# First-layer weights in five chunks: the 64 remaining features as high and low parts on both row halves

## The chip, the cores and the metric

The kernel runs on one core of a Trainium2 chip. The metric is the device time in microseconds, the median of several executions; lower is better. Inputs are made from a fixed seed and are float32.

## What is computed

An mLSTM-like recurrence over 4 batches, 8 heads, 768 steps and a head size of 40 is followed by two pairs of feed-forward layers on the 3072 x 320 result. Cut to what matters:

```python
x = attn_out.transpose(0, 2, 1, 3).reshape(B * S, H * D)     # 3072 x 320
def _moe_ref(x, w_in, w_out):        # w_in 320 x 2048, w_out 2048 x 320
    h = x @ w_in
    return np.maximum(0.01 * h, h) @ w_out
def _moe2_ref(x, w_in, w_out):       # the same shapes
    h = x @ w_in
    return (h * np.cos(h)) @ w_out
```

The change is in `h = x @ w_in`, in both pairs. Both products are made in three terms of rounded operands: with x = x_hi + x_lo and w = w_hi + w_lo, the kernel sums w_hi x_hi, w_hi x_lo and w_lo x_hi (for some features w_lo x_lo too).

## The kernel before

**Tiling.** The 3072 rows are 8 blocks of 384 (`BLOCKS`, `BLOCK`), half a batch each, three units of 128 rows in a block. The hidden size of 2048 is 16 tiles of 128 (`FT`). For each block and tile TensorE makes a first product (`first_product`, line 635 of the profile's numbering `L635`: eight matmuls of 128x384) and, three tiles later (`LAG`), a second product (`second_product`, lines 647 to 649: nine of 128x320). The first pair of layers runs over all 8 blocks, then the second pair.

**Stages in time.** Up to 36 us the first three units of the recurrence are computed with nothing beside them. From there on `slot(row, i)` of each engine is called for each tile i by `over_the_row`; into the slots of a block the steps of the next three units are put (`UNIT_SLOTS`, and `FIRST_SLOTS` for block 0: scores in slots 3, 7 and 11, probabilities one slot later, outputs two, read three, transposition four). Each engine executes its own list strictly in order, and the order is written out by hand; engines meet through semaphores (`wait_ge`, `then_inc`). From 480 us on the second pair of layers runs, with nothing of the recurrence beside it.

**The features.** 320 features are two chunks of 128 and a remainder of 64 (`REM`). The remainder fills a chunk of its own by standing twice, on partitions 0 to 63 and 64 to 127. In x (`xT`, five chunks) chunks 0 and 1 are the high parts of the full chunks, 3 and 4 their low parts; chunk 2 has the remainder's high part on the lower half of the partitions and its low part on the upper half. In the weights (`w_in`, six chunks) 0 to 2 are high parts and 3 to 5 low parts, the remainder's being the same on both halves. So the pair (weights 2, x 2) gives w_hi x_hi + w_hi x_lo of the remainder and (weights 5, x 2) gives w_lo x_hi + w_lo x_lo.

**Making the parts of x.** TensorE transposes a unit, ScalarE copies all three chunks in rounded form (`round_turned`), VectorE subtracts (`split_turned`, lines 1185 and 1186, called by `x_lo` for the first pair of layers and in `slot` under `turn2` for the second, into `stage`, which goes to DRAM and comes back).

**Making the parts of the weights.** SyncE loads raw pieces of two tiles (`load_raw_in`, two buffers, so that piece k waits for the splits of piece k-2), ScalarE rounds all three chunks (`split_in_hi`, `swap_in_hi`), and the rest is a subtraction: on GpSimd for pieces 0 and 1 (line 1447), on VectorE for pieces 2 to 7 (line 1283) in slots 1, 2, 5, 6, 9 and 10 of block 0 (`LATE_IN`). For the second pair of layers, GpSimd does it tile by tile during block 7 (`swap_in_lo`, line 1470), each followed by the output weights' rest (`swap_out_lo`, line 1476).

**The order around the start.** GpSimd: `split_in_lo(0)`, `second_columns()` (gate steps, lines 1435 and 1438, which wait for VectorE's scan `gate_decays(1)`, line 1051), `split_out_lo(0)` (line 1482), `split_in_lo(1)`, `split_out_lo(1)`, then unit 3. SyncE: raw piece 2 of both weights, the second of which waits for `split_out_lo(0)`, then the decays of units 3 and 4, then raw piece 3. VectorE at the end of the first stage: `normalised(0, 2)`, `gate_decays(1)`, `x_lo(0, 0)`, `outputs(0, 2)`, `x_lo(0, 1)`, `x_lo(0, 2)`.

Of the kernel before, what the change touches and what calls it, by code (L numbers as in the profile page):

```python
# [20 lines left out]
F32 = mybir.dt.float32  # L21
F32R = mybir.dt.float32r
ALU = mybir.AluOpType
ACT = mybir.ActivationFunctionType

P = 128
# [4 lines left out]
BLOCK = SEQ // HALVES  # L31
BLOCKS = BATCH * HALVES
TILES = BLOCK // P
DM, FF = HEADS * HD, 2048
FT = FF // P
REM = DM - 2 * P
SUB, SUBS = 64, 2
# [11 lines left out]
PIECES = 8  # L49
RAW_IN, RAW_OUT = 2, 2  # L50
# [3 lines left out]
PT = FT // PIECES  # L54
# [21 lines left out]
def build(nc, qk, q3, kvo, ig, fg, w1i, w1o, w2i, w2o, out, g_dram, e_dram, x2_dram):  # L76
    ctx = ExitStack()
    with ctx:
        def sb(name, shape, dt=F32):
            return ctx.enter_context(nc.sbuf_tensor(name, shape, dt))  # L80
# [4 lines left out]
        def sem(name):  # L85
            return ctx.enter_context(nc.semaphore(name))


        w_in = sb("w_in", [P, 6, FF], F32R)
        w_out = sb("w_out", [P, 2, FT, DM], F32R)  # L90
        raw_in = sb("raw_in", [P, RAW_IN, 3, PT * P])
        raw_out = sb("raw_out", [P, RAW_OUT, PT, DM])

        xT = sb("xT", [P, 2, 5, BLOCK], F32R)
        stage_f = sb("stage", [P, 5, BLOCK])
        stage = stage_f[:, :, :].bitcast(F32R)
        g_hi = sb("g_hi", [P, RING, BLOCK], F32R)
        g_lo = sb("g_lo", [P, RING, BLOCK], F32R)
# [63 lines left out]
        colb_done = sem("colb_done")  # L162
        win_hi = sem("win_hi")
        win_lo = sem("win_lo")
        wout_hi = sem("wout_hi")
        wout_lo = sem("wout_lo")
        arg_done = sem("arg_done")
# [91 lines left out]

        def half_cols(k):  # L260
            return slice(k * BLOCK, (k + 1) * BLOCK)

        def splits(k):

            return k + 1 if k < PIECES else PIECES + (k - PIECES + 1) * PT
# [80 lines left out]
        @block.sync  # L346
        def _(sp):
            sp.dma_start(f_s[:, half_cols(0)], fg[:, half_cols(0)]).then_inc(gates_in, 16)

            def wait_count(semaphore, count):  # L350
# [65 lines left out]

            load_qk(0, 0)
            sp.dma_start(f_s[:, half_cols(1)], fg[:, half_cols(1)]).then_inc(gates_in1, 16)
            sp.dma_start(i_s[:, half_cols(1)], ig[:, half_cols(1)]).then_inc(gates_in1, 16)
            load_kvo(0, 0)  # L420
            load_q3(0, 0)
# [119 lines left out]
        def _(pe):  # L541
# [88 lines left out]

            def first_product(bank, x, j):
                w = lambda k: w_in[:, k, j * P:(j + 1) * P]
                order = [(0, 0), (0, 3), (3, 0), (1, 1), (1, 4), (4, 1), (2, 2), (5, 2)]
                for n, (a, k) in enumerate(order):
                    last = nc.tensor.matmul(bank[:, 0:BLOCK], w(a), x[:, k, :], start=(n == 0), stop=(n == 7))  # L635
                last.then_inc(h_done, 1)
# [25 lines left out]
            def slot(row, i):  # L662
# [3 lines left out]
                if exists(row, i) and not row.in_mlp2(i):  # L666
                    if j == 0:
                        pe.wait_ge(xT_done, row.block(i) * TILES + TILES)
                    if row.starts(0, i) and j % PT == 0:
                        pe.wait_ge(win_lo, j // PT + 1)  # L670
                    pe.wait_ge(max_done, row.tile(i) - 1 + H_FREE)
                    first_product(h_bank[i % 2], xT[:, row.half(i)], j)
                elif exists(row, i):
                    if j == 0:
                        pe.wait_ge(x2_in[row.half(i)], row.block(i) * 8 - 8 * row.half(i) - 48)
                    if row.starts(BLOCKS, i):
                        pe.wait_ge(win_lo, PIECES + j + 1)
                        if j < H_FREE:
                            pe.wait_ge(max_done, row.tile(i) - 1 + H_FREE)
                    pe.wait_ge(prod_done, row.tile2(i) - 3 + PROD_FREE)  # L680
                    first_product(ring_bank[i % 4], xT[:, row.half(i)], j)
# [333 lines left out]
        def _(dve):  # L1015
            tt = nc.vector.tensor_tensor
# [164 lines left out]
            def split_turned(dst, bank, t):  # L1181

                r = slice(t * P, (t + 1) * P)
                src = bank[:, 0:3 * P].rearrange("p (a t) -> p a t", a=3)
                tt(dst[:, 3:5, r], src[:, 0:2, :], dst[:, 0:2, r].bitcast(F32), ALU.subtract)
                return tt(dst[REM:P, 2, r], src[REM:P, 2, :], dst[REM:P, 2, r].bitcast(F32), ALU.subtract)  # L1186

            def x_lo(b, c, dst):
                dve.wait_ge(xh_done, unit(b, c) + 1)
                split_turned(dst, turn_bank(b, c), c % TILES).then_inc(xT_done, 1)  # L1190
# [5 lines left out]
            def slot(row, i):  # L1196
# [41 lines left out]
                if t is not None:  # L1238
                    dve.wait_ge(x2_hi, (row.block(i) - 1) * TILES + t + 1)
                    split_turned(stage, x_bank, t).then_inc(x2_split, 1)  # L1240
                if row.starts(0, i) and i in LATE_IN:
                    split_in_lo(LATE_IN[i])
# [36 lines left out]
            def split_in_lo(k):  # L1279
                dve.wait_ge(win_hi, k + 1)  # L1280
                dve.wait_ge(win_lo, k)
                c = slice(k * PT * P, (k + 1) * PT * P)
                tt(w_in[:, 3:6, c], raw_in[:, k % RAW_IN, :, :], w_in[:, 0:3, c].bitcast(F32), ALU.subtract).then_inc(win_lo, 1)

            gate_maxima(1)
            first_probs(0)
# [27 lines left out]
        def _(pool):  # L1314
# [129 lines left out]
            def split_in_lo(k):  # L1444
                pool.wait_ge(win_hi, k + 1)
                c = slice(k * PT * P, (k + 1) * PT * P)
                nc.gpsimd.tensor_tensor(w_in[:, 3:6, c], raw_in[:, k % RAW_IN, :, :], w_in[:, 0:3, c].bitcast(F32),
                                        ALU.subtract).then_inc(win_lo, 1)

            def unit_weights(b, c):  # L1450
                if c == 0:
# [14 lines left out]
            def swap_in_lo(j):  # L1466

                pool.wait_ge(win_hi, PIECES + j + 1)
                k, c = PIECES + j // PT, slice(j * P, (j + 1) * P)
                nc.gpsimd.tensor_tensor(w_in[:, 3:6, c], raw_in[:, k % RAW_IN, :, j % PT * P:(j % PT + 1) * P],  # L1470
                                        w_in[:, 0:3, c].bitcast(F32), ALU.subtract).then_inc(win_lo, 1)

            def swap_out_lo(j):
                pool.wait_ge(wout_hi, PIECES + j + 1)
# [21 lines left out]
            second_inputs()  # L1496
            gated(0, 1)
            split_in_lo(0)
            second_columns()
            split_out_lo(0)  # L1500
            split_in_lo(1)
            split_out_lo(1)
            unit_weights(0, 3)
# [31 lines left out]
            for i in range(SWAP_IN, 2 * FT + 2):  # L1535
                if i >= FT + 2:
                    g_rest(0, i - FT - 2)
                if i < SWAP_IN + FT:
                    swap_in_lo(i - SWAP_IN)
                if SWAP_OUT <= i < SWAP_OUT + FT:  # L1540
                    swap_out_lo(i - SWAP_OUT)
# [58 lines left out]
```

## Time and profile before

| | |
|---|---|
| median of 3 executions | 835.13 us (834.86 to 835.85) |
| the profiled execution | 836.9 us, span 835.1 us |
| TensorE busy | 98% of the span |
| VectorE busy | 76% |
| ScalarE busy | 56% |
| GpSimd busy | 41% |
| mean granted clock of TensorE | 0.996 |
| DMA | 70.26 MB, mean 84 GB/s |

How to read it: the span runs from the first to the last instruction of the profiled execution, and that execution's own time is a little more. Busy shares are means over stages with different limits: a busy TensorE is where little can be hidden, and the idle time of the other engines costs nothing in itself. "Idle before, releaser" names what ended an engine's wait by the semaphores. The names: PE is TensorE, PEld its weight loads, DVE VectorE, ACT ScalarE, POOL GpSimd, SP SyncE.

### The profile page before, as it was taken

The numbers are of one execution on the slowest core, as the hardware profiler recorded it, in microseconds if no ns is written. First come the engines' busy times: TensorE is split into PE (matmuls) and PEld (weight loads), VectorE is DVE, ScalarE is ACT, GpSimd is POOL, SyncE is SP. The second block draws the span as 40 slices with busy tenths as digits, with TensorE's granted clock in tenths as the row PEclk, the third lists the DMA queues.
The fourth block names the chain that finished last, engine by engine and source line by source line (L and its number), as shares of the span: only waits on it lengthen the run. The fifth ranks groups of instructions, "written<-read, shape, count | busy, mean of one in ns | idle before, by whom it ended". The sixth has DMA issues, their size and how long they took to land.

```text
span 835.1 us, 18267 instructions
## 1 busy us (share of the span) xinstructions
PE 815.9 (98%) x6953; PEld 784.8 (94%) x6953; DVE 633.1 (76%) x1377; ACT 465.3 (56%) x1033; POOL 339.9 (41%) x350
## 2 busy tenths in 40 slices
PE   8789999999999999999999999999999999999997
PEld 6678899999999999999999999999999999999997
DVE  7679677677677866777853588888888888888886
ACT  5245443433433434334336687767776767777776
POOL 5656534343333433433316643333333333333332
PEclk9989999999999999999999999999999999999999
DMA  9555522423444324235023410302020202020000
GB/s 300 174 151 149 172 78 79 126 78 82 129 134 131 89 79 125 79 91 183 1 96 108 121 75 2 119 2 72 1 72 1 72 1 71 1 72 1 20 5 25
DMA packets 37292, 70.26 MB, mean 84 GB/s; under 512 B 3544, under 2 KB 24408, under 8 KB 37208
## 3 DMA queue, kind: packets, MB, share of 16 engines
q1 hardware_dynamic: 36708, 68.86, 26.7%
q8 instruction: 55, 0.90, 0.5%
q10 hardware_dynamic: 500, 0.26, 0.1%
q14 instruction: 29, 0.24, 0.1%
HBM read 57.11 MB, written 11.99 MB: 83 GB/s over the span
## 4 chain that ended last, share of the span: by engine, by line
PE 90%; DVE 4%; ACT 1%; DMA 1%; issue 1%; POOL 1%; SPq 1%; DVEq 0%; POOLq 0%; ACTq 0%
PE h L635 32%; PE acc L647 13%; PE acc L649 13%; PE acc L648 13%; PE s L635 10%; PE x L613 2%; PE s L593 2%; PE s L577 2%; PE s L605 2%; PE s L558 1%; DVE g_lo L1194 1%; DMA raw_in<-w1i 1%; DVE kvo_s L1073 1%; DMA eG_b<-e_dram 1%; ACT t_f L791 0%
## 5 line engine op out<-in xcount | busy, mean ns | idle before, releaser
L635 PE MATMUL h<-xT,w_in 128*128 128x384 f32 x1536 | 306.5, 341 | 0.5 <-DVE xT L1186 0.5
L635 PEld LDWEIGHTS h<-xT,w_in 128*128 128x128 f32 x1536 | 266.5, 188 | 3.6 <-DVE xT L1186 0.6
L791 ACT ACTIVATE t_f<-h 128x384 f32<-128x384 f32 x192 | 94.4, 492 | 291.9 <-PE h L635 291.8
L647 PE MATMUL acc<-w_out,g_hi 128*128 128x320 f32 x768 | 242.1, 315 | 2.2 <-POOL g_lo L1533 1.8
L649 PE MATMUL acc<-w_out,g_lo 128*128 128x320 f32 x768 | 237.5, 309 | 0.0
L648 PE MATMUL acc<-w_out,g_hi 128*128 128x320 f32 x768 | 236.2, 308 | 0.0
L1533 POOL TENSOR_TENSOR g_lo<-g_f,g_hi 128x384 fp32r<-128x384 f32 x127 | 130.2, 1025 | 211.9 <-ACT g_hi L791 211.9
L1207 DVE TENSOR_TENSOR g_f<-h,t_f 128x384 f32<-128x384 f32 x128 | 71.2, 556 | 105.7 <-ACT t_f L791 105.7
L647 PEld LDWEIGHTS acc<-w_out,g_hi 128*128 128x128 f32 x768 | 144.6, 188 | 4.6 <-POOL g_lo L1533 2.0
L648 PEld LDWEIGHTS acc<-w_out,g_hi 128*128 128x128 f32 x768 | 144.7, 188 | 0.0
L649 PEld LDWEIGHTS acc<-w_out,g_lo 128*128 128x128 f32 x768 | 144.3, 188 | 0.0
L791 ACT ACTIVATE g_hi<-g_f 128x384 fp32r<-128x384 f32 (+1 forms) x258 | 132.8, 515 | 1.6 <-DVE g_f L1227 1.0
L1219 DVE SCALAR_TENSOR_TENSOR r_f<-t_f,r_f 128x384 f32<-128x384 f32 x127 | 115.0, 906 | 4.4
L1380 POOL TENSOR_TENSOR Cm<-C,own 80x328 f32<-80x328 f32 x44 | 36.4, 830 | 170.2 <-DVE C L1175 140.5
L635 PE MATMUL s<-xT,w_in 128*128 128x384 f32 x512 | 100.8, 338 | 0.0
L1194 DVE TENSOR_TENSOR g_lo<-g_f,g_hi 128x384 fp32r<-128x384 f32 x128 | 95.7, 748 | 0.0
L635 PEld LDWEIGHTS s<-xT,w_in 128*128 128x128 f32 x512 | 89.7, 188 | 0.0
L1215 DVE TENSOR_SCALAR t_f<-t_f 128x384 f32<-128x384 f32 x127 | 46.8, 368 | 45.9 <-ACT t_f L791 45.8
L937 ACT ACTIVATE r_f<-r_f,half_pi 128x384 f32<-128x384 f32 x127 | 78.6, 619 | 4.1
L935 ACT ACTIVATE r_f<-r_f 128x384 f32<-128x384 f32 x127 | 65.5, 515 | 0.0
L1073 DVE RECIPROCAL kvo_s<-kvo_s 128x160 f32<-128x160 f32 x48 | 55.1, 1148 | 4.6 <-ACT kvo_s L791 4.5
L791 ACT ACTIVATE t_f<-s 128x384 f32<-128x384 f32 x64 | 31.6, 493 | 41.6 <-PE s L635 41.6
(150 smaller groups left out, 792.5 us busy)
## 6 DMA issues: line engine op xcount, KB each, us to landing
qk_s<-qk SPq DMA_DIRECT2D x24, 512.0 KB, 3.8
kvo_s<-kvo SPq DMA_DIRECT2D x24, 484.0 KB, 5.2
x_dram<-stage SPq DMA_DIRECT2D x8, 960.0 KB, 6.0
xT<-x_dram SPq DMA_DIRECT2D x8, 960.0 KB, 4.9
D<-g_dram SPq DMA_DIRECT2D x42, 128.0 KB
qe<-q SPq DMA_DIRECT2D x24, 160.0 KB, 5.5
out<-x SPq DMA_DIRECT2D x24, 160.0 KB, 1.8
eG_b<-e_dram SPq DMA_DIRECT2D x42, 80.0 KB
```

The costliest lines, as they stand in the source:

```text
L635: last = nc.tensor.matmul(bank[:, 0:BLOCK], w(a), x[:, k, :], start=(n == 0), stop=(n == 7))
L647: nc.tensor.matmul(acc[t][:, 0:DM], g_hi[:, s, r], w_out[:, 0, j, :], start=(j == 0), stop=False)
L648: nc.tensor.matmul(acc[t][:, 0:DM], g_hi[:, s, r], w_out[:, 1, j, :], start=False, stop=False)
L649: nc.tensor.matmul(acc[t][:, 0:DM], g_lo[:, s, r], w_out[:, 0, j, :], start=False, stop=(j == FT - 1)).then_inc(out_done, 1)
L791: copy = lambda o, i, **k: nc.scalar.activation(o, i, ACT.Copy, **k)
L935: nc.scalar.activation(r, r, ACT.Abs).then_inc(fold_done, 1)
L937: nc.scalar.activation(r, r, ACT.Sin, bias=half_pi[:, 0:1], scale=-1.0).then_inc(sin_done, 1)
L1073: nc.vector.reciprocal(o, o).then_inc(sig_done, 1)
L1194: tt(g_lo[:, i % RING, :], g_f[:, i % RING, :], g_hi[:, i % RING, :].bitcast(F32), ALU.subtract).then_inc(lo_done, 1)
L1207: tt(g_f[:, i % RING, :], h_bank[i % 2][:, 0:BLOCK], t_f[:, i % 2, :], ALU.max).then_inc(max_done, 1)
L1219: nc.vector.scalar_tensor_tensor(r, k, -TWO_PI_LO, r, ALU.mult, ALU.add).then_inc(red_done, 1)
L1533: nc.gpsimd.tensor_tensor(g_lo[:, s, :], g_f[:, s, :], g_hi[:, s, :].bitcast(F32), ALU.subtract).then_inc(lo_done, 1)
```

## The change

`w_in` has five chunks in place of six, `xT`, `stage` and `x2_dram` six in place of five. x now holds high parts in 0 to 2 and low parts in 3 to 5, the remainder's on both halves of the partitions. In the weights, chunk 2 has the high part of the remainder on one half and the low part on the other: for even tiles the low part is on the upper half (`rest_rows`), for odd tiles on the lower. So (weights 2, x 2) gives w_hi x_hi + w_lo x_hi, and (weights 2, x 5), in place of (weights 5, x 2), gives the products with x_lo. `split_turned` is one subtraction of three chunks. Each split of weights is a subtraction of two chunks and, for each tile, one of a half chunk in place. On GpSimd these wait for one another by a new semaphore `win_step`. ScalarE's steps are the same.

```diff
-        w_in = sb("w_in", [P, 6, FF], F32R)
+        w_in = sb("w_in", [P, 5, FF], F32R)
-        xT = sb("xT", [P, 2, 5, BLOCK], F32R)
-        stage_f = sb("stage", [P, 5, BLOCK])
+        xT = sb("xT", [P, 2, 6, BLOCK], F32R)
+        stage_f = sb("stage", [P, 6, BLOCK])
+        def rest_rows(j):
+            return slice(SUB * (1 - j % 2), SUB * (2 - j % 2))
@@ first_product
-                order = [(0, 0), (0, 3), (3, 0), (1, 1), (1, 4), (4, 1), (2, 2), (5, 2)]
+                order = [(0, 0), (0, 3), (3, 0), (1, 1), (1, 4), (4, 1), (2, 2), (2, 5)]
@@ split_turned (VectorE)
-                tt(dst[:, 3:5, r], src[:, 0:2, :], dst[:, 0:2, r].bitcast(F32), ALU.subtract)
-                return tt(dst[REM:P, 2, r], src[REM:P, 2, :], dst[REM:P, 2, r].bitcast(F32), ALU.subtract)
+                return tt(dst[:, 3:6, r], src, dst[:, 0:3, r].bitcast(F32), ALU.subtract)
@@ split_in_lo (VectorE)
-                tt(w_in[:, 3:6, c], raw_in[:, k % RAW_IN, :, :], w_in[:, 0:3, c].bitcast(F32), ALU.subtract).then_inc(win_lo, 1)
+                for j in range(PT):
+                    r, b = rest_rows(j), slice((k * PT + j) * P, (k * PT + j + 1) * P)
+                    tt(w_in[r, 2, b], raw_in[r, k % RAW_IN, 2, j * P:(j + 1) * P], w_in[r, 2, b].bitcast(F32), ALU.subtract)
+                tt(w_in[:, 3:5, c], raw_in[:, k % RAW_IN, 0:2, :], w_in[:, 0:2, c].bitcast(F32), ALU.subtract).then_inc(win_lo, 1)
@@ split_in_lo (GpSimd)
-                nc.gpsimd.tensor_tensor(w_in[:, 3:6, c], raw_in[:, k % RAW_IN, :, :], w_in[:, 0:3, c].bitcast(F32),
-                                        ALU.subtract).then_inc(win_lo, 1)
+                nc.gpsimd.tensor_tensor(w_in[:, 3:5, c], raw_in[:, k % RAW_IN, 0:2, :], w_in[:, 0:2, c].bitcast(F32),
+                                        ALU.subtract).then_inc(win_step, 1)
+                pool.wait_ge(win_step, PT * k + 1)
+                for j in range(PT):
+                    r, b = rest_rows(j), slice((k * PT + j) * P, (k * PT + j + 1) * P)
+                    nc.gpsimd.tensor_tensor(w_in[r, 2, b], raw_in[r, k % RAW_IN, 2, j * P:(j + 1) * P], w_in[r, 2, b].bitcast(F32),
+                                            ALU.subtract).then_inc(win_step if j == 0 else win_lo, 1)
+                    if j == 0:
+                        pool.wait_ge(win_step, PT * k + 2)
@@ swap_in_lo (GpSimd)
-                nc.gpsimd.tensor_tensor(w_in[:, 3:6, c], raw_in[:, k % RAW_IN, :, j % PT * P:(j % PT + 1) * P],
-                                        w_in[:, 0:3, c].bitcast(F32), ALU.subtract).then_inc(win_lo, 1)
+                r, b = rest_rows(j), slice(j % PT * P, (j % PT + 1) * P)
+                nc.gpsimd.tensor_tensor(w_in[:, 3:5, c], raw_in[:, k % RAW_IN, 0:2, b], w_in[:, 0:2, c].bitcast(F32),
+                                        ALU.subtract).then_inc(win_step, 1)
+                pool.wait_ge(win_step, PT * RAW_IN + j + 1)
+                nc.gpsimd.tensor_tensor(w_in[r, 2, c], raw_in[r, k % RAW_IN, 2, b], w_in[r, 2, c].bitcast(F32),
+                                        ALU.subtract).then_inc(win_lo, 1)
+                pool.wait_ge(win_lo, PIECES + j + 1)
@@ kernel
-    x2_dram = nc.dram_tensor("x2_dram", [BLOCKS, P, 5, BLOCK], F32, kind="Internal").ap()
+    x2_dram = nc.dram_tensor("x2_dram", [BLOCKS, P, 6, BLOCK], F32, kind="Internal").ap()
```

## Rows read from the trace of the kernel before

**Rows 1.** The page, part 1: TensorE's busy time, share of the span, instructions.

```profile
PE 815.9 (98%) x6953; PEld 784.8 (94%) x6953; DVE 633.1 (76%) x1377; ACT 465.3 (56%) x1033; POOL 339.9 (41%) x350
```

**Rows 2.** Windows: stretch, length, busy us by engine, granted clock, DMA share, GB/s.

```profile
52.00:54.00 2.00, 2.00 (x18) 1.85 (x19) 2.00 (x3) 0.00 (x0) 0.68 (x1) 0.50 0.14 27
...
57.40:57.60 0.20, 0.20 (x3) 0.20 (x2) 0.20 (x1) 0.20 (x1) 0.00 (x0) 0.83 0.00 0
...
300.00:400.00 100.00, 99.81 (x1036) 93.51 (x1035) 73.38 (x185) 41.16 (x99) 33.55 (x35) 1.00 0.38 116
```

**Rows 3.** TensorE's waits: who waited for whom, us in total, times, longest.

```profile
PE s L577 <- DVE D L1081: 4.5, 2, 3.4
...
PE x L613 <- DVE xT L1186: 0.4, 2, 0.2
```

**Rows 4.** The chain that ended last, 31 to 53 us: start, us, what.

```profile
31.87 0.85 DVE t_f L1051
32.79 0.99 POOL stage L1435
...
41.12 6.27 DMA raw_in<-w1i
...
48.30 0.96 DVE w_in L1283
...
51.91 1.38 PE s L577 x16
```

**Rows 5.** Timeline, TensorE, 45 to 47 us: start, length, engine, line, operation.

```profile
45.07 0.31 PE L649 MATMUL acc<-w_out,g_lo 128*128 128x320 f32 x1
...
45.22 0.31 PE L647 MATMUL acc<-w_out,g_hi 128*128 128x320 f32 x1
...
45.36 0.31 PE L648 MATMUL acc<-w_out,g_hi 128*128 128x320 f32 x1
...
45.51 1.38 PEld L635 LDWEIGHTS h<-xT,w_in 128*128 128x128 f32 x8
```

**Rows 6.** Timeline, VectorE and GpSimd, 29 to 34 us.

```profile
29.78 1.80 POOL L1447 TENSOR_TENSOR w_in<-raw_in,w_in 128x768 fp32r<-128x768 f32 x1
...
31.78 0.94 DVE L1051 TENSOR_TENSOR_SCAN t_f<-r_f,stage 32x384 f32<-32x384 f32 x1
32.64 0.39 DVE L1185 TENSOR_TENSOR xT<-x,xT 128x256 fp32r<-128x256 f32 x1
...
33.04 0.29 DVE L1186 TENSOR_TENSOR xT<-x,xT 64x128 fp32r<-64x128 f32 x1
...
33.37 0.18 DVE L1145 TENSOR_TENSOR x<-acc,kvo_s 128x24 f32<-128x24 f32 x1
```

**Rows 7.** Groups by line and shape: busy us, mean ns; idle before and releaser.

```profile
L1207 DVE TENSOR_TENSOR g_f<-h,t_f 128x384 f32<-128x384 f32 x128 | 71.2, 556 | 105.7 <-ACT t_f L791 105.7
...
L1470 POOL TENSOR_TENSOR w_in<-raw_in,w_in 128x384 fp32r<-128x384 f32 x16 | 16.4, 1024 | 29.4 <-ACT w_in L791 29.4
```

**Rows 8.** Timeline, VectorE and TensorE, 65 to 72 us.

```profile
65.78 2.60 DVE L1194 TENSOR_TENSOR g_lo<-g_f,g_hi 128x384 fp32r<-128x384 f32 x1
...
71.06 0.81 PE L577 MATMUL s<-kvo_s,kw 64*80 64x82 f32 x16 [1.14 <-DVE D L1081]
```

**Rows 9.** Timeline, GpSimd and VectorE, 42 to 46 us.

```profile
42.31 1.06 POOL L1351 TENSOR_TENSOR D<-D,colb 128x512 f32<-128x512 f32 x1 [2.35 <-DMA eG_b<-e_dram]
...
42.53 1.66 DVE L1283 TENSOR_TENSOR w_in<-raw_in,w_in 128x768 fp32r<-128x768 f32 x1
...
43.52 1.82 POOL L1356 TENSOR_TENSOR D<-D,hide 128x512 f32<-128x512 f32 x1
```

**Rows 10.** Timeline, GpSimd, 466 to 470 us, in the exchange of weights.

```profile
466.35 1.03 POOL L1470 TENSOR_TENSOR w_in<-raw_in,w_in 128x384 fp32r<-128x384 f32 x1 [0.86 <-ACT w_in L791]
...
467.34 0.87 POOL L1476 TENSOR_TENSOR w_out<-raw_out,w_out 128x320 fp32r<-128x320 f32 x1
```

**Rows 11.** The page, part 6: DMA issues, KB each, us to landing.

```profile
x_dram<-stage SPq DMA_DIRECT2D x8, 960.0 KB, 6.0
```

More of the change, by code:

```diff
@@ L164, in build @@
         win_lo = sem("win_lo")
+        win_step = sem("win_step")
         wout_hi = sem("wout_hi")
```

## The prediction
> **What bounds the kernel now.** I read the page first. TensorE is busy for 815.9 of 835.1 us [rows 1], so only what TensorE waits for, or what changes the pace of its own instructions, can move the time. The windows come next: from 300 to 400 us it is busy for 99.81 of 100 us at full clock [rows 2]. All that it loses is at the start, before the second layer products are in full flow, and at the very end. The list of TensorE's waits says who is to blame [rows 3]: 4.5 us in two places behind VectorE's `D` (the decayed scores), the longest 3.4 us, and 0.4 us in two places behind the low halves of x, line 1186. The chain that ended last tells how the first of these comes about [rows 4]. A scan on VectorE at 31.87 us releases GpSimd's gate steps at 32.79; behind them in GpSimd's order stands the rest of the first output weights, which lets SyncE go on to the loads of the decays, and only then, at 41.12, to the load of first-layer piece 3. That lands 6.27 us later, ScalarE rounds it, VectorE takes its rest at 48.30 (line 1283), and behind it, in VectorE's own order, come a maximum, a rest, a reciprocal and the product `D`, for which TensorE waits until 51.91. [...]
>
> **TensorE's own work.** Each of the 256 first-layer tiles keeps eight matmuls of 128x384. The last one was (weights 5, x 2) and is (weights 2, x 5). Nothing is removed and no shape changes, so I cost it at nothing. The only new thing is that the last two matmuls of a tile load the same weights. The trace has this already in the second layer: from line 649 to 647 the weights change and the step is 0.15 us, from line 647 to 648 they stay and it is 0.14 us [rows 5]. These are the same within the rounding.
>
> **The low halves of x (48 times, lines 1185 and 1186).** Two VectorE instructions become one. Before, they run from 32.64 to the next start at 33.37, 0.73 us [rows 6]. The one that takes their place is a 128x384 difference with one source in PSUM, as line 1207, 556 ns [rows 7]. The scan before them starts its successor 0.08 us before its own end (31.78 + 0.94 against 32.64) [rows 6], so the step should be 0.48 us: 0.25 us saved to the next instruction, and 0.33 + 0.40 - 0.56 = 0.17 us to the semaphore. TensorE waits for this in two places, in full 0.4 us, the longest 0.2 [rows 3]: 0.17 us each, together -0.35 us (bounds 0 and -0.4). The start of the first tile at 36.07 also comes earlier, but that gain flows into the 3.4 us wait behind it and is worth nothing.
>
> **The rests of the weights on VectorE (six pieces, line 1283).** One 128x768 instruction becomes two of 64x128 and one of 128x512. From 556 ns for 384 [rows 7] and 0.96 us for 768 [rows 4] an element costs 1.05 ns and the start 0.15 us; so 512 takes 0.69 us, and 64x128 takes 0.29 us, which is also what line 1186 shows for 64x128 [rows 6]. If each overlaps its successor by 0.08 us, the three take 0.21 + 0.21 + 0.61 = 1.03 us against 0.88, +0.15. Line 1186, on the upper half of the partitions, overlaps neither way (0.40 us from start to start for its neighbour of 0.39, then 0.33 for 0.29) [rows 6]; if both small ones behave so, it is 0.33 + 0.33 + 0.61 = 1.27, +0.39. I take +0.25, between these ends that lie near each other. This stands in the chain once, for the piece at 48.30. [...]
>
> **The rests on GpSimd at the start (pieces 0 and 1, line 1447).** One of 128x768, 1.80 us [rows 6], becomes 128x512, a wait on its own end, 64x128, a wait, 64x128. From 1024 ns for 384 [rows 7] an element costs 2.02 ns and the start 0.25 us: 1.28 + 0.51 + 0.51 us. A wait of GpSimd for its own instruction costs 0.15 us (42.31 + 1.06 against 43.52) [rows 9]. That is 2.6 us in place of 1.8, and piece 0 runs from 29.78 to 32.4. GpSimd has nothing to do before 32.79, so in itself this is hidden. But the scan that opens the chain starts at 31.78 and reads two tensors of SBUF [rows 6]. Such VectorE instructions and GpSimd's exclude each other in this trace: line 1283 at 42.53 takes 1.66 us instead of 0.96 beside GpSimd's `D` steps, and GpSimd's at 43.52 takes 1.82 for the same 512 elements for which 1.28 was worked out [rows 9]; line 1194 at 65.78 takes 2.60 us instead of some 0.55 [rows 8]. The second small one would start at 31.9, on top of the scan. If it waits for the scan, it runs until 33.2 and the gate steps start then instead of at 32.79; if the scan waits for it, the scan ends 0.5 us later. Both give about +0.4 us on the chain. Bounds: 0, if the scan is not touched, and +0.6. I take +0.40. Who waits: the gate steps, the output weights behind them, SyncE's queue and the load at 41.12. Piece 1 starts behind that chain and ends at some 39.2 us, when SyncE needs it only at 41.5: hidden. [...]
>
> **The second wait, 1.14 us at 71.06.** Ahead of it stand, on VectorE, a split of weights, line 1194 with its 2.60 us behind GpSimd, the x split and a reciprocal [rows 8]. The x split gives -0.25 us. The weight split has the blocked stretch after it as cover. Bounds: -1.14, if GpSimd and VectorE take turns better so that the wait goes away, and +1.3, if one of the three new instructions waits for one more GpSimd instruction (1.3 us is the price of 512 elements). I take -0.25.
>
> **The exchange of weights (16 tiles, line 1470).** Each 1.03 us becomes 128x256 (0.77) + 0.15 + 0.51 + 0.15 us = 1.6 us; with the output weights of 0.87 us it makes 2.5 us in a period of 2.7 (0.86 idle, then 0.99 to the next start, then 0.87) [rows 10]. [...] Its weights are needed a whole block later, so I cost it at 0; if GpSimd fell behind by 0.2 us in each of the 16, it would reach the next block's `g_lo` 3 us late, of which the lag of three tiles (8 us) hides all.
>
> **Transfers.** The stores and loads of x2 carry 6/5 of 960 KB, 1152 KB, landing about 1.2 us later than 6.0 us [rows 11]; each has more than a third of a block to land in. Nothing.
>
> **The sum** against the profiled execution (span 835.1, own time 836.9): +0.40 + 0.25 - 0.25 - 0.35 = +0.05 us. That execution lies 1.8 us above the median of 835.13, and the difference is put on the median: 835.2 us. The bounds are -1.14 - 0.4 + 0 + 0.15 = -1.4 us and 0.6 + 0.39 + 1.3 - 0 = +2.3 us.
>
> **Rivals.** [...] The first chain takes its upper ends (+0.99) and the second wait its own (+1.3, one of the three instructions of the split of weights ahead of it queues behind one more of GpSimd), while the two waits for x give back 0.35: +1.9 us, 837.1. It decides from the point where at least 1 us is lost at the second wait. For it speaks the 2.60 us of line 1194, against it that the stretch at 65.78 is blocked until 68.38 already, so that a delay of the split vanishes in it. 12 in 100. (b) Faster by the clock: the low-clock stretch after the wait costs half of 57.5 - 51.9, that is 2.8 us. If the wait moves so that the fall no longer comes, the time is 832.4. Against it: the wait gets longer in my sum, by 0.65 us and by TensorE's earlier start. 4 in 100. (c) Faster by the taking of turns: the second wait goes (-1.14), and the chain is not touched (0.15): 835.13 - 1.14 - 0.35 + 0.15 = 833.8, still within 0.2%, 8 in 100. [...] 3 in 100. (e) The longer wait also makes the low-clock stretch longer: half as long again is +1.4 us, with the first chain's +0.65 and -0.6 after it 836.6: within 0.2%, 6 in 100.
>
> **How the numbers follow.** The forecast itself has 67 in 100. 0.2% is 1.67 us, about what a measurement of this kernel can tell from no change. Within it lie the forecast, (c) and (e), 81 in 100; slower is (a), 12; faster are (b) and (d), 7. The range takes in (c) and (e) and most of (a): 833.6 to 837.0.
>
> **What would show it.** The gate step at 32.79 should start at 33.1 to 33.3 and the load of piece 3 at 41.5; the three instructions of the piece at 48.7 should take 1.0 to 1.3 us to the next start; TensorE's first long wait should end near 52.5, the second be shorter by a quarter of a microsecond, and the two waits for x's low halves be gone. TensorE's steps of 0.172 and 0.145 us should be as before. The forecast is wrong if these steps move, if the clock falls in another place, or if a wait appears in the blocks after 100 us.

## The result and the profile after

The changed kernel takes 837.36 us (median of 13), the one before 835.84 us beside it; the ratio is 1.0023, with a 95% interval of 1.0012 to 1.0033. It is slower by 1.9 us (1.0 to 2.8). I had forecast 835.2 us, that is no change against the 835.13 of before, and a range up to 837.0: a loss of 1.9 us was not in it. Of the 2.2 us between 835.2 and 837.36 some 0.7 belong to the kernel before, whose median is higher in this larger set of executions.

The two profiled executions hardly differ in span, 835.3 against 835.1 us, and this has to be cleared up first. The windows from 46 to 60 us, before first and after second, show why (columns as in [rows 2]):

```profile
46.00:60.00 14.00, 10.61 (x100) 9.86 (x100) 9.97 (x24) 6.03 (x12) 4.77 (x5) 0.76 0.56 153
```

```profile
46.00:60.00 14.00, 11.59 (x125) 10.62 (x126) 11.19 (x30) 6.48 (x14) 5.93 (x7) 0.88 0.62 161
```

Both lose clock at TensorE's long wait near 50 us (before is granted 0.50 from 51.0 to 57.4), but the execution of before that was profiled loses twice as much of it (granted 0.76 against 0.88). In time that is 3.4 us lost (0.24 of 14) against 1.7 (0.12 of 14). The other traces below show 0.76, 0.88 or 1.00 there, and neither the edits nor the length of the wait orders them. Executions of one and the same kernel differ by some 3 us, and this is part of it. So I compare stretches that lie behind it, from one landmark of TensorE's order to the next. The landmarks are waits that both traces have. After:

```profile
69.05 0.80 PE L582 MATMUL s<-kvo_s,kw 64*80 64x82 f32 x16 [0.64 <-DVE D L1086]
...
73.64 0.79 PE L598 MATMUL s<-Cm,qe 80*64 80x82 f32 x16 [0.88 <-POOL Cm L1387]
...
79.82 0.55 PE L618 MATMUL x<-ident,x 128*128 128x128 f32 x3 [0.45 <-DVE x L1154]
...
87.01 0.52 PE L582 MATMUL s<-kvo_s,kw 64*80 64x82 f32 x8 [1.80 <-DVE D L1086]
...
96.12 0.55 PE L618 MATMUL x<-ident,x 128*128 128x128 f32 x3 [0.99 <-DVE x L1154]
```

And the last of these landmarks before:

```profile
95.06 0.55 PE L613 MATMUL x<-ident,x 128*128 128x128 f32 x3 [0.99 <-DVE x L1149]
```

The first row answers to 71.06 in [rows 8]. From there to the last landmark it is 27.07 us after and 24.00 us before, 3.07 us more. From the last landmark to the end of the span it is 739.2 us after and 740.0 before, 0.9 us less. Together +2.2 us. Up to the first of these landmarks the changed kernel is 2.0 us ahead, 1.7 of it by the lesser loss of clock; the 0.3 us that are left bring the sum to +1.9 us, the measured loss. The new thing is the wait of 1.80 us at 87.01, where before had none worth naming.

What leads to it stands in the timeline of VectorE and GpSimd. Before, in the slots 9 to 12 of block 0:

```profile
80.01 1.42 POOL L1356 TENSOR_TENSOR D<-D,hide 128x512 f32<-128x512 f32 x1
81.38 1.45 POOL L1368 TENSOR_TENSOR kw<-kvo_s,colb 128x320 f32<-128x320 f32 x1
82.79 1.61 POOL L1362 TENSOR_TENSOR qe<-qe,eG_b 80x512 f32<-80x512 f32 x1
```

```profile
80.86 1.38 DVE L1283 TENSOR_TENSOR w_in<-raw_in,w_in 128x768 fp32r<-128x768 f32 x1
...
82.63 0.61 DVE L1194 TENSOR_TENSOR g_lo<-g_f,g_hi 128x384 fp32r<-128x384 f32 x1
```

After:

```profile
78.83 1.41 POOL L1363 TENSOR_TENSOR D<-D,hide 128x512 f32<-128x512 f32 x1
80.21 0.77 POOL L1375 TENSOR_TENSOR kw<-kvo_s,colb 128x320 f32<-128x320 f32 x1
80.94 1.95 POOL L1369 TENSOR_TENSOR qe<-qe,eG_b 80x512 f32<-80x512 f32 x1
82.85 1.56 POOL L1501 TENSOR_TENSOR w_out<-raw_out,w_out 128x640 fp32r<-128x640 f32 x1
```

```profile
79.80 1.32 DVE L1289 TENSOR_TENSOR w_in<-raw_in,w_in 64x128 fp32r<-64x128 f32 x2
81.05 0.68 DVE L1290 TENSOR_TENSOR w_in<-raw_in,w_in 128x512 fp32r<-128x512 f32 x1
...
82.12 2.70 DVE L1198 TENSOR_TENSOR g_lo<-g_f,g_hi 128x384 fp32r<-128x384 f32 x1
84.75 0.55 DVE L1190 TENSOR_TENSOR xT<-x,xT 128x384 fp32r<-128x384 f32 x1
...
86.27 0.68 DVE L1086 TENSOR_TENSOR D<-s,D 128x256 f32<-128x256 f32 x2
```

Read them as turns at one door; in the expectations I call it the port. What the rows show is who waits and for how long, not what the two engines share. The door concerns VectorE's instructions with two sources in SBUF: `g_f` (line 1207 before, 1211 after), with one source in PSUM, takes 0.54 to 0.56 us each of the 128 times, also at 81.65 in the middle of `qe`. Before, the single weight instruction is served behind GpSimd's `D`, `kw` waits for it (1.45 us in place of some 0.75), then the rest of g (`g_lo`, line 1194 before and 1198 after) is served between `kw` and `qe`. After, the first small one is served behind `D`, then GpSimd's `kw` comes at once (0.77 us), then the second small one and the large one, and it is `qe` that waits (1.95 us). The rest of g now asks at 82.12, while `qe` runs, and it isn't served at the end of `qe` at 82.89 but only at the end of the output weights' rest at 84.41. It takes 2.70 us instead of 0.61, and behind it in VectorE's order stand the x split, a reciprocal and the product `D` for which TensorE waits.

TensorE's own steps are as forecast. After, at full clock:

```profile
48.02 0.31 PE L652 MATMUL acc<-w_out,g_hi 128*128 128x320 f32 x1
48.16 0.31 PE L653 MATMUL acc<-w_out,g_hi 128*128 128x320 f32 x1
48.31 0.31 PE L654 MATMUL acc<-w_out,g_lo 128*128 128x320 f32 x1
```

The steps are those of [rows 5]; a matmul of the first layer takes 341 ns in the mean on the pages of both kernels. From 300 to 400 us TensorE is busy for 99.95 us with 1038 instructions against 1036 [rows 2].

### The profile page after: what moved, and what is told of

It reads as the page before. It is cut to its first block, busy times and chain, and to the rows that moved or that the text cites. A ratio compares the mean times of both kernels' runs of the same rounds, so it can differ in the third digit from the quotient of the medians.

```text
span 835.3 us, 18267 instructions
## 1 busy us (share of the span) xinstructions
PE 816.5 (98%) x6953; PEld 784.9 (94%) x6953; DVE 630.2 (75%) x1341; ACT 465.0 (56%) x1033; POOL 343.7 (41%) x370
## 4 chain that ended last, share of the span: by engine, by line
PE 90%; DVE 5%; ACT 2%; issue 1%; DMA 1%; POOL 0%; DVEq 0%; POOLq 0%; ACTq 0%
PE h L640 32%; PE acc L652 13%; PE acc L654 12%; PE acc L653 12%; PE s L640 10%; PE x L618 2%; PE s L598 2%; PE s L582 2%; PE s L610 2%; PE s L563 1%; DVE kvo_s L1078 1%; DVE g_lo L1198 1%; DMA eG_b<-e_dram 1%; DVE g_f L1211 1%; DMA raw_in<-w1i 0%
## 5 line engine op out<-in xcount | busy, mean ns | idle before, releaser
L1198 DVE TENSOR_TENSOR g_lo<-g_f,g_hi 128x384 fp32r<-128x384 f32 x128 | 97.9, 765 | 0.0
```

The lines of the kernel that those rows point to most:

```text
L1198: tt(g_lo[:, i % RING, :], g_f[:, i % RING, :], g_hi[:, i % RING, :].bitcast(F32), ALU.subtract).then_inc(lo_done, 1)
```

## The experiments

Every figure in us against the kernel before is the ratio's, on runs side by side on one chip.

**The parts of the change, one at a time.** VectorE's weight splits alone:

```diff
-                tt(w_in[:, 3:6, c], raw_in[:, k % RAW_IN, :, :], w_in[:, 0:3, c].bitcast(F32), ALU.subtract).then_inc(win_lo, 1)
+                for j in range(PT):
+                    r, b = rest_rows(j), slice((k * PT + j) * P, (k * PT + j + 1) * P)
+                    tt(w_in[r, 2, b], raw_in[r, k % RAW_IN, 2, j * P:(j + 1) * P], w_in[r, 2, b].bitcast(F32), ALU.subtract)
+                tt(w_in[:, 3:5, c], raw_in[:, k % RAW_IN, 0:2, :], w_in[:, 0:2, c].bitcast(F32), ALU.subtract).then_inc(win_lo, 1)
```

> Only the VectorE weight splits of the change: pieces 2 to 7 take two instructions of 64x128 and one of 128x512 in place of one of 128x768. x keeps five chunks, the last matmul of a tile repeats (weights 2, x 2), chunk 5 goes unread, so the products of the remainder are not the reference's. Theory 1 (port queue): 1.5 to 2.8 us slower than before, and in the trace a new wait of TensorE of 1 us or more near 87 us behind line 1194's rest, itself of 2.5 us or more. Rival (the three instructions cost only their own length, +0.25 us on the first chain): 0.2 to 0.4 us slower and no new wait between 80 and 90 us.

Measured: 839.61 us against 835.55, ratio 1.0055 (1.0040 to 1.0070), +4.6 us. The wait near 87 us is 2.28 us long and from the first landmark to the last it is 27.06 us. Theory 1 holds for the wait and the rest of g ahead of it, 2.71 us, not for the price, of which I had expected 1.5 to 2.8 us. The part costs more than the whole change, by five executions; 3.1 of the 4.6 us lie between the landmarks, and where the rest lies was not settled.

The GpSimd weight splits alone (`split_in_lo` and `swap_in_lo` of GpSimd as in the diff of the change):

> Only the GpSimd weight splits of the change: pieces 0 and 1 at the start and the 16 tiles of the exchange are cut into their parts with the waits between. VectorE's splits stay single, x keeps five chunks, the last matmul of a tile repeats (weights 2, x 2), chunk 5 goes unread, so the products of the remainder are not the reference's. Theory 1: within 0.5 us of before; the scan at 31.8 us is lengthened by 0.2 us at most 0.5, which reaches the first long wait, and nothing is seen near 480 us. Rival (the start chain carries the loss): 1 us or more slower, with the first long wait of TensorE ending 1 us later.

Measured: 835.16 against 835.55 us, ratio 0.9999 (0.9988 to 1.0010). From landmark to landmark 23.99 us, to the end 740.0 us: nothing. The chain at the start doesn't carry the loss.

The x part alone (`split_turned` in one instruction, six chunks; the weights' rests in single instructions into chunks 0 to 2):

> Only the x part of the change: x in six chunks, one VectorE subtraction of 128x384 for two, 1152 KB to and from DRAM. The weights' rests are single subtractions of three chunks as before, but take the place of the high parts in chunks 0 to 2, and the eight matmuls of a tile use these three chunks only, so the products are not the reference's. Theory 1 (the whole loss lies in VectorE's three small weight instructions): 0.9 to 1.9 us faster than before, with TensorE's waits for the low halves of x (0.2 us at 207 and 318 us) gone and 0.9 to 1.0 us less between 96 us and the end, as the changed kernel has it. Rival (x gives only the 0.35 us of my sum): 0.2 to 0.5 us faster.

Measured: 834.60 against 835.68 us, ratio 0.9992 (0.9978 to 1.0005). The interval holds both no gain and 1.8 us; the trace says more:

```profile
70.23 0.81 PE L582 MATMUL s<-kvo_s,kw 64*80 64x82 f32 x16 [0.66 <-DVE D L1086]
...
74.80 0.79 PE L598 MATMUL s<-Cm,qe 80*64 80x82 f32 x16 [0.86 <-POOL Cm L1384]
...
94.60 0.55 PE L618 MATMUL x<-ident,x 128*128 128x128 f32 x3 [0.99 <-DVE x L1154]
```

To the end of the span (833.7) it is 739.1 us from the last landmark, 0.9 less than before, as in the changed kernel. The first row has the wait of 1.14 us [rows 8] shortened by 0.5 us, and the second shows where that goes: the next wait grows from 0.37 to 0.86 us. Larger transfers cost nothing.

**Which piece.** VectorE's splits as in w_vector_only, but for the last piece (`if k < 7:`), and then for the last piece alone (`if k == 7:`):

> As w_vector_only, but the last piece (slot 10 of block 0) has its single 128x768 subtraction back; the products of the remainder are not the reference's. Theory 1 (one starved rest at slot 10 carries most of the loss: GpSimd takes the port for the small instructions' sake one instruction earlier, and the rest of tile 9 then waits through two of GpSimd's in a row): the wait of TensorE near 87 us falls from 2.3 to under 0.3 us, and the time from 4.1 to some 1.5 to 2 us above before. Rival (each of the six pieces costs its share by the length of its instructions): the loss falls by a sixth, to some 3.4 us.

Measured: 836.42 against 835.68 us, ratio 1.0010 (1.0001 to 1.0019); 23.93 us between the landmarks, no wait at 83 us. Five pieces in three instructions cost 0.8 us, less than the 1.5 to 2 I had expected, and by difference the sixth 3.8. The stall one unit earlier is still there, 2.71 us for line 1198 at 63.66 as in before at 65.78, and TensorE's second wait is 2.00 us in this trace, whose clock did not fall.

> The kernel before, but VectorE's last piece of weights alone (piece 7, slot 10 of block 0) is taken in three instructions; x keeps five chunks, the last matmul of a tile repeats (weights 2, x 2), so the products of the remainder are not the reference's. Theory 1 (the piece at slot 10 shifts the turn at the port, and one starved rest costs the time): a wait of TensorE of 1.5 to 2.3 us near 87 us, nothing of it at the other pieces, and 2 to 3 us slower than before. Rival (the six pieces add up, or the stall needs the shifts of the pieces before it): 0 to 0.6 us slower and no such wait.

Measured: 838.57 against 835.39 us, ratio 1.0037 (1.0022 to 1.0053), +3.1 us; 26.7 us between the landmarks. Its rows:

```profile
83.29 2.71 DVE L1198 TENSOR_TENSOR g_lo<-g_f,g_hi 128x384 fp32r<-128x384 f32 x1
```

```profile
88.67 0.52 PE L581 MATMUL s<-kvo_s,kw 64*80 64x82 f32 x8 [2.31 <-DVE D L1085]
```

One piece in one slot is the loss. The rival, that pieces add up, has fallen: the other five together cost 0.8 us (0.1 to 1.6) against 3.1 (1.8 to 4.4).

**Fewer small instructions.** The low part on the upper half for every tile, one 64x256 in a piece:

```diff
-            return slice(SUB * (1 - j % 2), SUB * (2 - j % 2))
+            return slice(SUB, P)
@@ VectorE
+                tt(w_in[SUB:P, 2, c], raw_in[SUB:P, k % RAW_IN, 2, :], w_in[SUB:P, 2, c].bitcast(F32), ALU.subtract)
```

> The changed kernel with the low part of the remainder on the upper half for every tile, so that the two small instructions of a piece are one of 64x256: two VectorE instructions in a piece in place of three, two on GpSimd at the start. Theory 1 (each small instruction may queue anew, and shifts GpSimd's turn): the same stall near 87 us, if one small instruction is enough to shift the turn, and then at most 0.5 us faster than the changed kernel; without the stall 2 us faster or more. Rival (number of instructions counts): 0.2 us in each of the pieces on the path, 0.5 us in all.

Measured: 837.16 against 835.68 us, ratio 1.0014 (1.0001 to 1.0027). The stall is there, 2.69 us and a wait of 1.74 us at 87 us. One instruction more than before is enough to shift the turn.

**Opening the door.** GpSimd waits for its own `qe` ahead of the output weights' rest:

```diff
             unit_weights(0, 3)
+            pool.wait_ge(qe_done, 4)
             split_out_lo(2)
@@ and in units 4 and 5 alike
```

> The changed kernel, with one wait more on GpSimd in each of units 3, 4 and 5: for the end of its own product qe, ahead of the output weights' rest, so that GpSimd has an idle moment between the two. Theory 1 (the rest of g on VectorE is starved because GpSimd passes from qe, on 80 partitions, into the next instruction without letting the port go): the 2.6 and 2.7 us instructions of line 1198 near 64 and 82 us fall to 1.6 us or less, the waits of TensorE near 69 and 87 us go, and the time falls by 2 to 3 us, to 0.5 us or more below before. Rival (GpSimd keeps its turn whatever the gap): no change against the changed kernel.

Measured: 835.92 against 835.68 us, ratio 1.0000 (0.9987 to 1.0014), about 1.9 us less than the changed kernel has over before, but not the 0.5 us below before that I had expected. GpSimd and VectorE:

```profile
78.47 1.95 POOL L1369 TENSOR_TENSOR qe<-qe,eG_b 80x512 f32<-80x512 f32 x1
80.50 1.77 POOL L1501 TENSOR_TENSOR w_out<-raw_out,w_out 128x640 fp32r<-128x640 f32 x1
```

```profile
79.65 1.19 DVE L1198 TENSOR_TENSOR g_lo<-g_f,g_hi 128x384 fp32r<-128x384 f32 x1
...
83.36 1.67 DVE L1198 TENSOR_TENSOR g_lo<-g_f,g_hi 128x384 fp32r<-128x384 f32 x1
```

The rest of g asks at 79.65, during `qe`, as in the changed kernel, and is done at 80.84: it enters in the 0.08 us between `qe` and the next. The waits at 69 and 87 us shrink to nothing and 0.31 us. Part of the gain is missing because another wait appears, 1.50 us at 87.98: the next rest of g (second row) now finds the next output weights in its way. The granted clock may take another part: of the twelve executions six have a mean of 0.998 and take 833.3 to 834.9 us, six have 0.991 to 0.994 and take 837.0 to 838.4, so that the median of 835.92 lies between two groups. The kernel before has 0.997 in the mean of its 35, this one 0.996. What takes the clock in the second group wasn't traced.

> The kernel before with the same three waits on GpSimd as in after_gap. Its rest near 66 us takes 2.60 us behind two GpSimd instructions, and TensorE waits 1.14 us at 71 us. Theory 1: this falls to 1.6 us or less, the wait goes, and the time falls by 0.7 to 1.5 us. Rival (the turn at the port does not depend on the gap): no difference.

Measured: 833.92 against 835.39 us, ratio 0.9991 (0.9974 to 1.0007), -0.8 us: not settled by the times. In the trace the rest of g falls from 2.60 us [rows 8] to 1.07, and TensorE has no wait over 0.12 us between 53 and 93 us. The stall was in the kernel before too, at unit 4, and I had read it as given.

> The changed kernel with one small instruction of 64x256 in a piece (as paired2) and the three waits on GpSimd of after_gap. Theory 1: as after_gap or up to 0.4 us faster, since one start less stands in each piece, and 0.5 to 1.5 us below before by the saving on x. Rival (the gap helps only together with a certain place of the small instructions): as paired2.

Measured: 835.79 against 835.39 us, ratio 1.0003 (0.9994 to 1.0012), as after_gap; the 0.5 to 1.5 us below before did not come. Its trace has the same new wait, 1.60 us at 88.38.

**How long the door stays shut behind `qe`.** First `kw` and `qe` in the other order:

```diff
-                keys(b, c)
-                carried(b, c)
+                carried(b, c)
+                keys(b, c)
```

> The changed kernel with GpSimd's kw (128 partitions) and qe (80 partitions) in the other order in every unit, so that the instruction ahead of the output weights' rest is the one on 128 partitions, still with no wait between. [...] Theory 1b (any two GpSimd instructions with no wait between keep the port): the stalls stay, within 0.5 us of the changed kernel.

Measured: 837.86 against 835.39 us, ratio 1.0029 (1.0017 to 1.0041).

```profile
80.92 1.33 POOL L1369 TENSOR_TENSOR qe<-qe,eG_b 80x512 f32<-80x512 f32 x1
82.22 0.72 POOL L1375 TENSOR_TENSOR kw<-kvo_s,colb 128x320 f32<-128x320 f32 x1
82.90 1.56 POOL L1501 TENSOR_TENSOR w_out<-raw_out,w_out 128x640 fp32r<-128x640 f32 x1
```

```profile
80.52 4.08 DVE L1289 TENSOR_TENSOR w_in<-raw_in,w_in 64x128 fp32r<-64x128 f32 x2
84.53 0.68 DVE L1290 TENSOR_TENSOR w_in<-raw_in,w_in 128x512 fp32r<-128x512 f32 x1
```

The time is what theory 1b gives (0.5 us more than the changed kernel, within the noise), the rows are not so simple. I had expected VectorE to be served behind `kw`, since that uses all 128 partitions, and the time to fall by 1.5 to 3 us. It is not: the second small instruction now waits through `qe`, `kw` and the output weights, and ends at 84.61. But theory 1b falls by the rows of before above, where VectorE is served between `kw` and `qe` with no wait between (0.61 us at 82.63). What fits both is that VectorE stays shut out behind `qe` for more than one instruction. So the same order with a wait behind `qe` and none behind `kw`:

```diff
                 carried(b, c)
+                if isinstance(b, int) and b == 0:
+                    pool.wait_ge(qe_done, unit(b, c) + 1)
                 keys(b, c)
```

> after_swap with one wait more in units 3 to 5: GpSimd waits for the end of qe (80 partitions) before kw (128 partitions); between kw and the output weights' rest there is still no wait. [...] Theory 1b (any two GpSimd instructions with no wait between keep the port): the small ones are served in the gap, but the rest of line 1198 waits for kw and the output weights' rest both, 2.2 us or more.

Measured: 835.54 against 835.74 us, ratio 0.9999 (0.9989 to 1.0010), 2.5 us less against before than after_swap.

```profile
79.21 1.33 POOL L1369 TENSOR_TENSOR qe<-qe,eG_b 80x512 f32<-80x512 f32 x1
80.62 1.26 POOL L1375 TENSOR_TENSOR kw<-kvo_s,colb 128x320 f32<-128x320 f32 x1
81.84 1.88 POOL L1503 TENSOR_TENSOR w_out<-raw_out,w_out 128x640 fp32r<-128x640 f32 x1
```

```profile
78.79 1.90 DVE L1289 TENSOR_TENSOR w_in<-raw_in,w_in 64x128 fp32r<-64x128 f32 x2
...
81.68 0.61 DVE L1198 TENSOR_TENSOR g_lo<-g_f,g_hi 128x384 fp32r<-128x384 f32 x1
```

The small ones are served in the gap, `kw` waits for them, and the rest of g at 81.68 is served between `kw` and the output weights, with no wait there. Theory 1b has fallen: the rest of g takes 0.61 us and not the 2.2 or more that it gives. So far the rule would be that the door stays shut behind `qe`, on 80 partitions, until GpSimd has waited for its own end: the two small ones take 4.08 us without that wait and 1.90 with it. One case in after_swap limits it, in unit 3:

```profile
45.84 1.34 POOL L1369 TENSOR_TENSOR qe<-qe,eG_b 80x512 f32<-80x512 f32 x1
47.15 1.37 POOL L1375 TENSOR_TENSOR kw<-kvo_s,colb 128x320 f32<-128x320 f32 x1
51.05 1.54 POOL L1501 TENSOR_TENSOR w_out<-raw_out,w_out 128x640 fp32r<-128x640 f32 x1 [2.54 <-ACT w_out L796]
```

```profile
44.75 2.58 DVE L1289 TENSOR_TENSOR w_in<-raw_in,w_in 64x128 fp32r<-64x128 f32 x2
47.26 0.67 DVE L1290 TENSOR_TENSOR w_in<-raw_in,w_in 128x512 fp32r<-128x512 f32 x1
```

GpSimd doesn't wait between `qe` and `kw` here either, and yet the second small one, which starts at 46.05 and takes 1.28 us, is done at 47.33, 0.15 us after the end of `qe`, and `kw` is the one that waits (1.37 us in place of 0.72). What stands behind `kw` differs from unit 5: here the output weights start only at 51.05, after a wait of 2.54 us for ScalarE, there they follow at once, at 82.90. So the work that is ready behind `qe` is the 0.72 us of `kw` here, and VectorE was served ahead of it; in unit 5 of after_swap it is 2.3 us (0.72 and 1.56), in the changed kernel 1.56 us (the output weights), and VectorE was served behind it. That is one case against the others. Whether the length of the ready work decides, no run shows.

Nor do the runs show why the door stays shut. No run changed the number of partitions of `qe` alone; for it as the condition speaks that in before the `D` step on 128x512 at 80.01, 1.42 us long, lets VectorE in with no wait behind it (line 1283, 1.38 us at 80.86).

**A version that beats both.** after_gap, and the second output weights in units 4 and 5 wait for VectorE's rest of that slot:

```diff
             split_out_lo(3)
+            pool.wait_ge(lo_done, 8)
             split_out_lo(4)
...
             split_out_lo(5)
+            pool.wait_ge(lo_done, 12)
             split_out_lo(6)
```

> after_gap with two waits more on GpSimd: the output weights' rests that come second in units 4 and 5 start only when VectorE has made the rest of the tile of that slot. In after_gap one of them stood 1.56 us in the way of line 1198 at 83.4 us and TensorE waited 1.51 us at 88 us for the chain behind it. Theory 1: that wait goes to under 0.3 us and the time falls by 1.0 to 1.6 us against after_gap, to 834.0 to 834.9, below before by 0.8 to 1.8 us. Rival (the later start of the output weights becomes a wait of its own): as after_gap or slower, with a wait of TensorE for the output weights of tiles 12 and 13 near 92 us.

Measured: 833.83 against 835.74 us, ratio 0.9983 (0.9973 to 0.9993), 1.4 us below before (0.6 to 2.3) and 3.3 us below the changed kernel by the two ratios.

```profile
82.44 0.52 PE L582 MATMUL s<-kvo_s,kw 64*80 64x82 f32 x8 [0.29 <-DVE D L1086]
...
86.27 0.79 PE L598 MATMUL s<-Cm,qe 80*64 80x82 f32 x16 [0.38 <-POOL Cm L1387]
...
91.58 0.55 PE L618 MATMUL x<-ident,x 128*128 128x128 f32 x3 [0.99 <-DVE x L1154]
```

The wait of 1.50 us is down to 0.38, not under the 0.3 I expected, and 739.1 us follow the last landmark. The gain against after_gap, 1.4 us, is in the range expected.

## Why the prediction was wrong, step by step

- **TensorE's own work: right.** No step moved: 0.14 and 0.15 us in the second layer, 341 ns for a matmul of the first.
- **The low halves of x: right in kind, mis-sized.** The one instruction takes 0.52 to 0.56 us into `xT` and 0.47 to the next start (0.48 worked out). I let only the two waits of [rows 3] pay, -0.35 us; behind 96 us it gives -0.9, in all kernels that have it, and in none of those that keep the two instructions. What each place pays was right, how many pay was wrong. Against before, TensorE gets ahead in five steps of 0.14 to 0.19 us, at 151.8, 207.3, 262.6, 318.1 and 373.5 us of before, each time at the transpositions of line 613. TensorE's matmuls name two of these waits; its weight loads, in the same list of before, name five:

```profile
PEld x L613 <- DVE xT L1186: 2.0, 5, 0.5
```

  At the second wait it gave -0.5 us where I had -0.25, and the next wait took it back.
- **VectorE's splits: this is the step that failed.** I had each piece cost its own length, once on the chain at 48.30 (+0.25 us), and looked for a wait behind GpSimd only at the piece ahead of the second wait. The piece at slot 10 costs 3 us: it lets GpSimd's `kw` go ahead, the rest of g then asks during `qe` and waits 2.70 us. I had weighed it among the covered ones without reading the rows around it. In before the rest of g asks at 82.63, 0.2 us before `kw` ends, and is let in; at 65.78 it asks 0.6 us into `qe` and is not. That small margin was what the cut used up.
- **The length of a piece: nearly right.** Where nothing of GpSimd's is in the way (after_gap at 47.17) the three instructions take 1.11 us to the next start against 0.88, +0.23, and the instruction before the first one loses its overlap of 0.08 besides, which my +0.25 left out. On the first chain the first small one meets `qe` (0.76 us at 47.04) and the three take 1.58 us, not 1.0 to 1.3.
- **Rival (a), the first, named the cause,** an instruction of VectorE's that queues behind one more of GpSimd's once the weights' rest is cut, and its price, 837.1 us, is near the measured 837.36. That nearness is luck: it had +0.99 on the first chain, +1.3 at the second wait and -0.35 for x, where the traces have +3.07 behind the second wait and -0.9 for x. It had the wrong place (the second wait; there the trace shows 0.64 us, shorter than before), and 12 in 100 was too little. What I held against it, that the stretch at 65.78 is blocked already, is true of that place only.
- **The range.** My bounds were -1.4 and +2.3 us, which on 835.2 is 833.8 to 837.5; the range that I gave ended at 837.0, below this upper bound and below rival (a)'s own 837.1.
- **GpSimd at the start: covered.** The second small one met the scan as worked out:

```profile
31.34 0.98 POOL L1459 TENSOR_TENSOR w_in<-raw_in,w_in 64x128 fp32r<-64x128 f32 x2
33.21 0.99 POOL L1442 TENSOR_TENSOR stage<-stage,t_f 32x384 f32<-32x384 f32 x1 [0.89 <-DVE t_f L1056]
```

  The scan took 1.14 us against 0.94 [rows 6], +0.2 where I took +0.4. The gate steps start 0.42 us later, of which 0.22 is there at the start of the scan already. The load of piece 3, issued at 42.12 and not at the 41.5 that I expected, landed in 4.0 us, against 6.27 [rows 4]. TensorE's first long wait is 2.30 us and not 3.39 and ends at 51.36, where I had expected 52.5. w_gpsimd_only, whose time does not change, is the better evidence that the start is covered.
- **The exchange: right.** Each tile takes GpSimd 0.75 and 0.46 us and two gaps of 0.08, less than I had; it idles 0.49 us in each period, and no wait comes of it.
- **The transfers: right.** 1152 KB land in 6.7 us.
- **The trade of time for profile.** I put the sum on the median, as the rows allowed. The profiled execution of before lost more clock at 50 to 57 us than most of the other traces; the sum, made of differences, did not need this.

## What to carry to other kernels

What cutting a VectorE instruction in three cost here was not its starts (+0.23 us where nothing of GpSimd's was in the way) but the new turns at the door: 3.1 us for one piece (w_vector_7alone), since they moved which later instruction had to wait. Where VectorE and GpSimd share a stretch, look at every place where the cut stands, and ask for each VectorE instruction with two SBUF sources behind it which GpSimd instruction it will meet. Where VectorE stands at the door behind a GpSimd instruction on part of the partitions, try a wait for that instruction's end: here one behind `qe`, on 80 partitions, in each of three units was worth 1.9 us in the changed kernel, while in the kernel before its 0.8 us are not told from nothing. When reading which waits a saving will shorten, read the weight loads' waits too: of five places that paid 0.17 us each, the matmuls' list named two.

## What the runs showed of the hardware that I had not expected

- Behind GpSimd's `qe` on 80 partitions, with 1.56 us or more of further GpSimd work ready, VectorE's instruction with two SBUF sources was not served until GpSimd had waited for its own end or was through with that work: 2.60 us (before, at 65.78), 2.70 (the changed kernel, at 82.12) and 2.71 (w_vector_7alone, at 83.29) for 0.55 us of work, and 4.08 us for two of 0.29 (after_swap, at 80.52). With 0.72 us ready it was served at the end of `qe` (after_swap, unit 3, one case). Behind `kw` on 128 partitions it was served with no wait between (0.61 us in before at 82.63 and in after_swap_gap at 81.68), but not behind the `kw` that followed `qe` at once in unit 5 of after_swap.
- A gap of 0.08 us on GpSimd was enough to be served in: behind `qe` in after_gap, where the rest of g takes 1.19 us at 79.65 in place of 2.70, and in after_swap_gap.
- TensorE's clock around its first long wait, of 1.3 to 3.9 us, was granted at 0.76, 0.88 or 1.00 in the mean from 46 to 60 us without regard to the edit: 0.76 with 3.39 us in before, 0.88 with 3.44 us in paired_gap. The wait of 2.30 us in w_vector_not7 lost no clock at all, that of 2.30 us in the changed kernel did.
